# Attention's turning product: three products of fp32r halves in place of one of plain fp32

## The reference, cut to what matters

```python
# q, k, v: (4, 8, 576, 64); all arithmetic is fp32
scores = scale * np.matmul(q, k.transpose(0, 1, 3, 2))
ret = scores * Dmat[None, :, :, :]          # gamma[h] ** (i - j) where i >= j, else 0
attn_out = np.matmul(ret, v)                # (4, 8, 576, 64)
x = attn_out.transpose(0, 2, 1, 3).reshape(4, 576, 512)
logits = np.einsum('bsd,de->bse', x, w_gate)                          # 8 columns
local_gate = 1 / (1 + np.exp(-np.einsum('bsd,de->bse', x, w_local)))  # 1 column
# each token goes through the expert of its largest logit, or, where
# local_gate >= 0.5, through the expert of the token before it
```

## Time and profile before

| | us |
|---|---|
| three runs: median, lowest, highest | 746.54, 746.21, 748.17 |
| span of the profiled execution, first to last instruction | 747.5 |
| TensorE busy in it | 679.3 (91%) |
| ScalarE, VectorE, GpSimd busy | 220.4 (29%), 283.2 (38%), 362.9 (49%) |
| turning product (line 638), 96 of them, 2 records each | 46.1 busy |

### The profile page before, as it was taken

One profiled execution on the slowest core, in us unless ns is written; L12 is line 12 of the kernel. 1 busy time (PEld: TensorE's weight loads), 2 busy tenths in 40 slices (PEclk: granted clock), 3 DMA queues, 4 the chain that ended last, 5 costly groups with the idle time before them and its releaser, 6 DMA issues.

```text
span 747.5 us, 14448 instructions
## 1 busy us (share of the span) xinstructions
PE 679.3 (91%) x4248; PEld 548.6 (73%) x4249; DVE 283.2 (38%) x594; ACT 220.4 (29%) x505; POOL 362.9 (49%) x226
## 2 busy tenths in 40 slices
PE   3999599935997799999999999948999999999998
PEld 2677377724786588888888888736987988988886
DVE  2656365672223033333233222327264065057031
ACT  1445245501222022222222222225433334234211
POOL 3656246223356999999999969457020011000000
PEclk9999799966999799999999999979999999999999
DMA  9999959208883344434443433232011002100101
GB/s 259 276 279 259 234 152 261 81 16 53 139 277 110 112 149 145 140 126 141 135 152 133 140 127 100 71 107 68 1 53 61 14 14 77 35 0 9 54 1 64
DMA packets 69493, 86.51 MB, mean 116 GB/s; under 512 B 14480, under 2 KB 42768, under 8 KB 69456
## 3 DMA queue, kind: packets, MB, share of 16 engines
q1 hardware_dynamic: 51040, 62.57, 30.1%
q0 software_dynamic: 3472, 11.28, 6.9%
q10 hardware_dynamic: 14944, 12.24, 5.0%
HBM read 70.06 MB, written 16.01 MB: 115 GB/s over the span
## 4 chain that ended last, share of the span: by engine, by line
PE 78%; DMA 9%; DVE 4%; issue 4%; POOL 3%; ACT 1%; POOLq 0%; DVEq 0%; ACTq 0%
PE ps L705 24%; PE ps L695 23%; DMA xg<-x_rows,slot_token 6%; PE ps L638 5%; PE ps L597 4%; PE ps L696 3%; PE ps L693 3%; PE ps L608 3%; PE ps L739 2%; PE ps L626 2%; PE ps L702 2%; PE ps L621 2%; PE ps L706 2%; DMA consts_sb<-constants 2%; DMA x_rows<-x_sb 1%
## 5 line engine op out<-in xcount | busy, mean ns | idle before, releaser
L531 POOL TENSOR_TENSOR w_lo<-stage,w_hi 128x1024 f32 x48 | 115.0, 2395 | 8.0 <-POOL w_hi L529 7.8
L529 POOL TENSOR_TENSOR w_hi<-stage,zero 128x1024 f32 x48 | 92.6, 1928 | 5.2 <-PE ps L706 5.2
L695 PE MATMUL ps<-w_lo,w_hi 128*128 128x288 f32 (+2 forms) x272 | 94.3, 347 | 0.0
L485 POOL TENSOR_TENSOR q_blocks<-q_in,consts_sb 64x576 f32<-64x576 f32 x32 | 44.9, 1402 | 67.5 <-PE ps L626 55.2
L705 PE MATMUL ps<-w_lo,xt_hi 128*128 x184 | 74.2, 403 | 0.0
L705 PE MATMUL ps<-w_lo,ht_hi 128*128 x184 | 72.7, 395 | 0.0
L695 PE MATMUL ps<-w_hi,w_lo 128*128 128x512 f32 (+2 forms) x204 | 70.7, 346 | 0.0
L695 PE MATMUL ps<-w_hi 128*128 128x512 f32 (+2 forms) x204 | 70.6, 346 | 0.0
L1239 DVE TENSOR_TENSOR xt_lo<-ps,xt_hi 128x512 fp32r<-128x512 f32 x25 | 17.3, 692 | 130.2 <-ACT xt_hi L948 120.5
L961 ACT CAST ht_hi<-ps 128x512 fp32r<-128x512 f32 x50 | 27.0, 590 | 126.9 <-PE ps L739 119.7
L705 PE MATMUL ps<-w_hi,ht_lo 128*128 x161 | 63.7, 395 | 0.0
(11 more groups left out here) (176 smaller groups left out, 1484.4 us busy)
## 6 DMA issues: line engine op xcount, KB each, us to landing
stage<-in_w SPq DMA_DIRECT2D x64, 512.0 KB, 3.5
y_slots<-y_sb ACTq DMA_DIRECT2D x25, 256.0 KB
q_in<-in_q_t SPq DMA_DIRECT2D x16, 288.0 KB, 4.4
kn_in<-in_k_n SPq DMA_DIRECT2D x16, 288.0 KB, 6.3
k_in<-in_k_t SPq DMA_DIRECT2D x16, 288.0 KB, 6.1
v_in<-in_v_n SPq DMA_DIRECT2D x16, 288.0 KB, 7.8
x_rows<-x_sb ACTq DMA_DIRECT2D x16, 288.0 KB, 5.8
out<-out_sb SPq DMA_DIRECT2D x16, 256.0 KB, 2.0
```

The source lines that it names most:

```text
L485: nc.gpsimd.tensor_tensor(q_blocks[d, u, h, :].rearrange("p (c t) -> p c t", c=NC), q_in[d, u, :].rearrange("p (c t) -> p c t", c=NC), q_d ...
L529: nc.gpsimd.tensor_tensor(hi, stage[:, j % HP, :], zero[:, 0:1].broadcast_to([P, PIECE]), ALU.add).then_inc(hi_done, 1)
L531: nc.gpsimd.tensor_tensor(lo, stage[:, j % HP, :], hi.bitcast(F32), ALU.subtract).then_inc(split_done, 1)
L695: nc.tensor.matmul(to, *p, start=False, stop=False)
```

## The change: what it does, and the diff

The 10 gate columns (9, and one of zeros so that the count is even) and the identity are kept as fp32r halves: `gate_hi` (138 columns) and `gate_lo` (10 columns; an identity has no rest). ScalarE's copy of `out_ps` now rounds to `xo_hi`, and VectorE has one new operation in each step, `out_lo`: `xo_lo` = `out_ps` minus `xo_hi`. The turning product becomes three, which add up in one place: `xo_hi` x `gate_hi` (138 columns), `xo_lo` x `gate_hi` (138), `xo_hi` x `gate_lo` (10). What waited for ScalarE's copy on TensorE (`out_copied`) now waits for VectorE's new operation (`out_split`). The identity is loaded once, and ScalarE copies it four times beside the gate columns, ahead of the loop.

```diff
-    ident_gate = place("ident_gate", [P, HP, P + G], F32)
+    GE = G + G % 2
+    gate_sb = place("gate_sb", [P, HP, GE], F32)
+    gate_hi = place("gate_hi", [P, HP, P + GE], F32R)
+    gate_lo = place("gate_lo", [P, HP, GE], F32R)
...
-    x_turned = place("x_turned", [P, 2, C], F32)
+    xo_hi = place("xo_hi", [P, 2, C], F32R)
+    xo_lo = place("xo_lo", [P, 2, C], F32R)
...
 def output(i, b2, hp, c):
-                pe.wait_ge(out_copied, n * NC + c + 1)
+                pe.wait_ge(out_split, n * NC + c + 1)
...
 def turn_and_logits(i, b2, hp, c):
-                pe.wait_ge(out_copied, n * NC + c + 3)
+                pe.wait_ge(out_split, n * NC + c + 3)
                 pe.wait_ge(rows_copied, n * NC + c + 1)
-                nc.tensor.matmul(turn_ps, x_turned[:, k, :], ident_gate[:, hp, :]).then_inc(turned, 1)
+                nc.tensor.matmul(turn_ps, xo_hi[:, k, :], gate_hi[:, hp, :], start=True, stop=False, skip_group_check=True)
+                nc.tensor.matmul(turn_ps, xo_lo[:, k, :], gate_hi[:, hp, :], start=False, stop=False, skip_group_check=True)
+                nc.tensor.matmul(turn_ps[:, P:P + GE], xo_hi[:, k, :], gate_lo[:, hp, :],
+                                 start=False, stop=True, skip_group_check=True).then_inc(turned, 1)
...
 # ScalarE, ahead of its loop
+            act.wait_ge(gate_zero, 1)
+            act.dma_start(gate_sb[:, :, 0:E], w_gate.rearrange("(k p) e -> p k e", p=P)).then_inc(gate_in, 16)
+            act.dma_start(ident[:, :], consts_dram[:, 0:P]).then_inc(ident_in, 16)
             act.wait_ge(decays_in, 16)
-            act.dma_start(ident_gate[:, :, 0:P], consts_dram[:, 0:P].rearrange("p (a e) -> p a e", a=1)
-                          .broadcast_to([P, HP, P])).then_inc(gate_in, 16)
+            act.wait_ge(ident_in, 16)
+            nc.scalar.copy(gate_hi[:, :, 0:P], ident[:, :].rearrange("p (a e) -> p a e", a=1).broadcast_to([P, HP, P])).then_inc(ident_cast, 1)
...
-                    nc.scalar.copy(x_turned[:, c % 2, :], out_ps[:, c % 2, :]).then_inc(out_copied, 1)
+                    nc.scalar.copy(xo_hi[:, c % 2, :], out_ps[:, c % 2, :]).then_inc(out_copied, 1)
...
 # VectorE
+            def out_lo(i, b2, hp, c):
+                n, k = pair(i, b2, hp), c % 2
+                dve.wait_ge(out_copied, n * NC + c + 1)
+                nc.vector.tensor_tensor(xo_lo[:, k, :], out_ps[:, k, :], xo_hi[:, k, :].bitcast(F32),
+                                        ALU.subtract).then_inc(out_split, 1)
...
                     if m + 1 < len(steps):
                         mask(i, *steps[m + 1])
+                    if m:
+                        out_lo(i, *steps[m - 1])
                     if c < NC - 1:
                         update_state(i, b2, hp, c)
```

More of the change, by code:

```diff
@@ L281, in build @@
         out_ps = ps[:, 3:5, 0:C]
-        turn_ps = ps[0:C, 5, 0:P + G]
+        turn_ps = ps[0:C, 5, 0:P + GE]
         state_ps = ps[:, 6, 0:DH]
@@ L287, in build @@
         gate_in = sem("gate_in")
+        gate_zero = sem("gate_zero")
+        gate_split = sem("gate_split")
+        gate_lo_done = sem("gate_lo_done")
+        ident_in = sem("ident_in")
+        ident_cast = sem("ident_cast")
+        out_split = sem("out_split")
         qk_in = [sem(f"qk_in{u}") for u in range(2)]
@@ L633, in turn_and_logits @@
                 k = c % 2
-                pe.wait_ge(out_copied, n * NC + c + 3)
+                pe.wait_ge(out_split, n * NC + c + 3)
                 pe.wait_ge(rows_copied, n * NC + c + 1)
                 if hp == 0 and c == 0:
-                    pe.wait_ge(gate_in, 64)
-                nc.tensor.matmul(turn_ps, x_turned[:, k, :], ident_gate[:, hp, :]).then_inc(turned, 1)
+                    pe.wait_ge(gate_lo_done, 1)
+                    pe.wait_ge(ident_cast, 1)
+                nc.tensor.matmul(turn_ps, xo_hi[:, k, :], gate_hi[:, hp, :], start=True, stop=False, skip_group_check=True)
+                nc.tensor.matmul(turn_ps, xo_lo[:, k, :], gate_hi[:, hp, :], start=False, stop=False, skip_group_check=True)
+                nc.tensor.matmul(turn_ps[:, P:P + GE], xo_hi[:, k, :], gate_lo[:, hp, :],
+                                 start=False, stop=True, skip_group_check=True).then_inc(turned, 1)
             with pe.Fori(0, B // 2) as i:
@@ L889, in _ @@
         def _(act):
-            act.dma_start(ident_gate[:, :, P:P + E], w_gate.rearrange("(k p) e -> p k e", p=P)).then_inc(gate_in, 16)
-            act.dma_start(ident_gate[:, :, P + E:P + G], w_local.rearrange("(k p) e -> p k e", p=P),
+            act.wait_ge(gate_zero, 1)
+            act.dma_start(gate_sb[:, :, 0:E], w_gate.rearrange("(k p) e -> p k e", p=P)).then_inc(gate_in, 16)
+            act.dma_start(gate_sb[:, :, E:G], w_local.rearrange("(k p) e -> p k e", p=P),
                           allow_slow_non_contiguous=True).then_inc(gate_in, 16)
+            act.dma_start(ident[:, :], consts_dram[:, 0:P]).then_inc(ident_in, 16)
             act.wait_ge(decays_in, 16)
             act.dma_start(consts[:, DECAYS - P:NCONST - P], consts_dram[:, DECAYS:NCONST]).then_inc(consts_in, 16)
-            act.dma_start(ident_gate[:, :, 0:P], consts_dram[:, 0:P].rearrange("p (a e) -> p a e", a=1)
-                          .broadcast_to([P, HP, P])).then_inc(gate_in, 16)
-            act.dma_start(ident[:, :], consts_dram[:, 0:P]).then_inc(gate_in, 16)
-            act.sem_inc(out_copied, 2)
+            act.wait_ge(ident_in, 16)
+            nc.scalar.copy(gate_hi[:, :, 0:P], ident[:, :].rearrange("p (a e) -> p a e", a=1).broadcast_to([P, HP, P])).then_inc(ident_cast, 1)
             act.sem_inc(rows_copied, 1)
@@ L915, in rows_of @@
                     act.wait_ge(logits_added, n + 1)
-                nc.scalar.copy(x_sb[:, u, c, :], turn_ps).then_inc(rows_copied, 1)
+                nc.scalar.copy(x_sb[:, u, c, :], turn_ps[:, 0:P + G]).then_inc(rows_copied, 1)
                 if c == NC - 1:
@@ L1052, in _ @@
             dve.sem_inc(s_read, 1)
+            dve.sem_inc(out_split, 2)
+            nc.vector.memset(gate_sb[:, :, :], 0.0).then_inc(gate_zero, 1)
             nc.vector.memset(zero[:, :], 0.0)
@@ L1057, in _ @@
             dve.wait_ge(zeroed, 1)
+            dve.wait_ge(gate_in, 32)
+            nc.vector.tensor_copy(gate_hi[:, :, P:P + GE], gate_sb[:, :, :]).then_inc(gate_split, 1)
+            dve.wait_ge(gate_split, 1)
+            nc.vector.tensor_tensor(gate_lo[:, :, :], gate_sb[:, :, :], gate_hi[:, :, P:P + GE].bitcast(F32),
+                                    ALU.subtract).then_inc(gate_lo_done, 1)
             dve.wait_ge(consts_in, 16)
@@ L1115, in _ @@
                         add_logits(i, *steps[m - NC][:2])
+                out_lo(i, *steps[-1])
                 add_logits(i, *steps[-1][:2])
```

## The result

| | before | changed |
|---|---|---|
| median of the runs, us | 746.38 (745.24 to 748.17, 4 runs) | 832.74 (831.64 to 834.78, 4 runs) |
| span of the profiled execution | 747.5 | 832.7 |

The changed kernel takes 1.116 times as long (95% interval 1.112 to 1.120), 86 us more. Slower was the forecast, but by 10 us, with 762 as the upper end: the size is wrong by a factor of nine, and so is the reason for most of it.

What follows compares the result with a forecast made beforehand. TensorE, busy throughout the steady attention stretch at full clock, was taken as the bound; 747.5 + 0.9 + 7.0 + 2.2 - 0.3 = 757.3, less 1.0 for span against median, gave 756 us, own range 753 to 760, 8-in-10 range 750 to 762.

Steps and rivals of the forecast that it cites:

- TensorE's part: Attention's turning product on TensorE: three short products in place of one, scores at 0.32 for 0.31 us, +0.9 us in sum.
- the five cases: Whole kernel: the forecast of 756 us and four alternatives at 748.3, 743.6, 763 and 750 us.
- The product's own size: Turning product on TensorE: +0.01 us in each of 96 steps, +0.9 us, bounds -10.6 to +4.8.
- Rival A: Turning products on TensorE: second to fourth loads hidden, -0.11 us x 96 = -10.6, total 748.3 us; chance 0.09.
- VectorE's stalls: Turning product waits for VectorE's new operation: +0.55 us at c = 2 (7.0 in sum), +0.14 at c = 4 (2.2).
- rival D: VectorE at c = 2: stalls move the weights clear of k_dec, 16 x 0.05 in place of 7.0, 750 us; chance 0.10.
- The gain of 0.3 us at the starts: Both loop turns: ScalarE's table load goes ahead of the loop, at most 0.4 us gained, taken as -0.3.
- the -1 to +1 that I had for the loads: Early loads of identity and gates: 256 KB less, taken as 0 us with bounds -1 to +1.
- my ±3: Hole where the loop turns: VectorE's 6.46 us of "issue" left as it is, bounds -3 to +3 us.
- The chance of slower: Whole kernel: slower by more than the 0.3% (2.2 us) a measurement can tell, chance 0.87.

Runs made afterwards that it cites:

- experiment 5: Changed kernel with 22 dense 512-column fp32r products into an unused bank between steps 6 and 7 of each loop turn: 767.9 us.
- 6: Changed kernel without VectorE's new operation and its wait, the second product taking xo_hi again: 834.3 us.
- experiment 4: Kernel before with the plain fp32 turning product cut to its last 72 columns in all but the first step: 817.1 us.
- 2: Changed kernel with one more plain fp32 product of 64 columns behind the turning products of each step, into an unused bank: 872.2 us.
- 7: Changed kernel with one more plain fp32 product of 512 columns right behind the scores in each step, into an unused bank: 823.7 us.
- 9: Changed kernel with dense products where TensorE waits, 14 at each turn's head and 16 ahead of the first output product: 764.4 us (1.024).
- 1: Changed kernel with 14 dense fp32r products of 512 columns ahead of TensorE's loop, into an unused bank: 838.7 us.
- experiment 3: Kernel before, turning product still plain fp32, with VectorE's new operation in each step and TensorE waiting for it: 753.0 us (1.008).
- the last run: Changed kernel with two turning products, dense blocks where TensorE waits, weights' rest in halves and xo_lo ahead of it: 744.5 us (0.994).

## Why the prediction was wrong

**The step that failed** is in TensorE's part: the new products are priced at 2.4 GHz ("So 138 columns take 0.06 us", a load 0.08), and everything around them is left at that level. I took the level of the kernel before, as given, a property of the stage. The runs show that it hangs on the products in the step. In my ranges for the products, -10.6 to +4.8 us, the level was not a term, and none of the five cases had it, though two rows in front of me did: the earlier trace rows has the loads of the first turning product at 0.40 us where they are 0.24 in the steady stretch (61.11 us), and the earlier trace rows has 0.50 for the routing. The kernel before spends its first steps at 1.2 GHz and gets out of it. Whether the changed one does was the question.

What the runs show: the full step costs 2.42 against 1.35 at the two levels (experiment 5, one run, same step). The level is lost for the whole of attention with the three products and without VectorE's part (6), and until 210 us with a single shorter product of plain fp32 (4). It is not given back by the same count of columns with one more seen load (2), but by many columns behind a hidden load (7), and by a dense block, after which the changed steps hold it (5, 9). What in a step decides stays open: no run varies one such thing alone, and the clock rose once at the start of the changed kernel (18.5 us, 5) and once late in steps that had run at 1.2 GHz (210 us, 4). What is shown is the effect: with the new products TensorE mostly stays at the level at which it starts, and a busy share of 100% does not tell that it does. The Trainium skill, in "TensorE: Matmul & The Clock Gate", section "What's actually happening", has the idle state at half the clock and activity as what releases it; the trace agrees in direction, with the clock rising within the dense block at 10.3 us and falling in the idle time behind it (1). That the engine is busy is not enough here: in the changed kernel it is busy for 76.66 us of 76.66 and the clock does not rise. I read that page for a rule against the change, and took the one on the gap between products in place of the one on the clock.

**The product's own size** was nearly right, in part by luck. With the level held, the full step is 1.35 in place of 1.33: +0.02 us where I had +0.01, some 2 us in 96 steps in place of 0.9. But from the turning product to the scores are 0.28 us (118.82 to 119.10, experiment 5), less than the 0.32 that I had, and from the scores to the state products 0.47 in place of 0.41, a price that my sum did not have. That three loads one behind the other set the pace shows at 1.2 GHz too: from the second product to the third are 0.16 us (61.16 to 61.32), twice the 0.08 of a load at 2.4 GHz and more than the 138 columns (0.115). Rival A, hidden loads with the scores 0.2 behind, is not what happened. (My lower bound for VectorE's operation, 200 ns, is not a third of the 692 that stand there, which is 231; nothing hangs on it.)

**VectorE's stalls** were right in kind and place, too large in sum. Expected +0.55 at c = 2 and +0.14 at c = 4; measured 0.38 and 0.15 in experiment 3, 0.34 and 0.13 in 5. The new operation takes 0.24 us and the hand-over 0.05, as said. The difference at c = 2 is that the stalls push the weights back against k_dec: they started 1.07 us behind its start (63.42 to 62.35) in place of 0.90, and took 1.02 us in place of 1.19. That is rival D, in part. In sum experiment 3 was 5.8 us longer where 9.2 were expected; that is what the stalls cost less what the shorter hole gave back, the second turn alone having lost 3.9. In the changed kernel itself they hardly exist: in its whole trace the turning product waits twice for xo_lo, 1.0 us in sum.

**The start and the turn.** The gain of 0.3 us at the starts did not come: the first turning product is 2.2 us later, outside the -1 to +1 that I had for the loads. The first scores, of the kernel before and of the changed one:

```profile
11.40 2.23 PE L597 MATMUL ps<-q_blocks,k_in 128*96 128x192 f32 x6 [11.40 <-POOL q_blocks L485]
...
13.92 2.23 PE L607 MATMUL ps<-q_blocks,k_in 128*96 128x192 f32 x6 [13.92 <-DMA v_in<-in_v_n]
```

They start at 13.3 to 14.7 us in all nine profiles with the changed kernel as base and at 11.1 to 12.2 in all five with the kernel before, so it belongs to the change; why the inputs come later was not tried. The hole became 4.0 us shorter, outside my ±3. VectorE's "issue" in it, which I had left at 6.46 us, is 2.63 in the changed kernel, 3.8 less:

```profile
130.50 0.62 DVE L1087 TENSOR_TENSOR probs<-ps,consts_sb 96x192 f32<-96x192 f32 x2 [2.63 <-issue]
```

The hole is as short in experiment 4 (7.3), at 1.2 GHz with the loop of before, and 11.3 in experiment 5, whose first turn ran at 2.4 GHz with the changed loop; which speaks for the pace of the turn and against the size of the loop; neither was tried by itself. The stages behind attention took between 590.8 and 597.6 us in the fourteen profiles, 590.8 to 596.9 with the kernel before as base and 591.9 to 597.6 with the changed one, so that the 4.4 us are no more than they vary by.

**The rivals.** None of the five was the case. The chance of slower, 0.87, was right mostly by luck: the reason given for it explains a tenth of what was measured.

## What to carry to other kernels

Before trading plain fp32 passes for short fp32r products, look whether the kernel before has slow steps at its start: they show that the stage has to earn its clock, which a product made cheaper on paper can cost it, whatever its operand type. Afterwards compare the length of a product that the change does not touch. Time such a change also with the level held by a dense block, which separates the price of the change from that of the level: in the two turns the change costs 8.1 us at 2.4 GHz, of the products and VectorE's stalls, against 91.5 in the changed kernel as it ran. An operation that TensorE waits for may stand better ahead of the long ones on its engine than behind them (744.5 against 749.7), but it moves the wait and does not remove it.

## What the runs showed of the hardware that I had not expected

- TensorE can be busy without a gap for 76.66 us at 1.2 GHz, and the same step holds 2.4 GHz once it is there (1.35 us for 54 us on end, experiment 5).
- The profile's granted clock reads 1.00 ahead of the first change on record (1.00 in a stretch where the scores' records are 614 ns, not 326). The lengths of known products decide.
- VectorE's subtraction of two SBUF tiles hardly proceeds beside GpSimd's k_dec: started while it runs, 512 columns end 0.55 us behind its end, whenever they started (59.85 to 59.30 in the kernel before, 64.44 to 63.89 in experiment 3, 54.88 to 54.33 in the last run), and 256 end 0.28 behind it; alone they take 0.69 and 0.41. Meanwhile xo_lo, which reads PSUM and one SBUF tile, took 0.24 to 0.26 throughout, also while k_dec ran (62.74 in experiment 3). The Trainium skill, in "SBUF — State Buffer", section "Who interferes with whom", says that a VectorE instruction with two SBUF inputs contends with a GpSimd one that reads SBUF, and that one with at most one SBUF input, outside the modes that use two ports, does not; the trace agrees.
